# Start of an attention and mixture-of-experts kernel: where the rows of sums are made, how a third slot gets its constant rows, and when a gate split is issued

## The reference

```python
# attention: batch 2, heads 8, sequence 576, head size 64
scores = scale * q @ k.T
cum = cumsum(maximum(s, 0))
bias = -(cum[..., :, None] - cum[..., None, :])
scores = where(causal, -1e9, scores + minimum(bias, 0))
attn = softmax(scores);  x = attn @ v            # -> 1152 tokens x 512
# mixture 1: top 2 of 8 experts, noisy gate; h = relu(x @ w1[e]); out += weight * h @ w2[e]
# mixture 2: all 8 experts, weights balanced by 8 row/column normalisations
```

## Time and profile before

| | us |
|---|---|
| median of 3 runs | 1206.88 (1205.94 to 1207.20) |
| the profiled execution, its own time | 1204.84 |
| its span, first to last instruction | 1203.1 |
| PE busy | 1188.2 |
| mean granted clock | 0.993 |

### The profile page before, as it was taken

One profiled execution on the slowest core, in us unless ns is written; L12 is line 12 of the kernel. 1 busy time (PEld: TensorE's weight loads), 2 busy tenths in 40 slices (PEclk: granted clock), 3 DMA queues, 4 the chain that ended last, 5 costly groups with the idle time before them and its releaser, 6 DMA issues.

```text
span 1203.1 us, 20068 instructions
## 1 busy us (share of the span) xinstructions
PE 1188.2 (99%) x7085; PEld 1062.0 (88%) x7085; DVE 697.3 (58%) x1584; ACT 426.4 (35%) x918; POOL 254.8 (21%) x303
## 2 busy tenths in 40 slices
PE   8999999999999999999999999999999999999998
PEld 6999888888888888889889899899899898898997
DVE  6664775554444451657566575575574675665753
ACT  7675344444344241224123232242241241332320
POOL 8767111111111456201001011011010010110110
PEclk9998999999999999999999999999999999999999
DMA  7770654444455420013120220210211201202102
GB/s 179 182 173 4 246 179 153 155 150 153 180 180 203 161 61 1 1 36 106 36 71 6 64 70 0 70 40 30 70 35 35 70 24 46 70 0 70 35 1 78
DMA packets 40230, 102.81 MB, mean 85 GB/s; under 512 B 4750, under 2 KB 23694, under 8 KB 38010
## 3 DMA queue, kind: packets, MB, share of 16 engines
q1 hardware_dynamic: 33722, 85.70, 22.7%
q0 software_dynamic: 3360, 11.01, 3.0%
q10 hardware_dynamic: 3104, 5.54, 1.4%
HBM read 87.82 MB, written 10.30 MB: 82 GB/s over the span
## 4 chain that ended last, share of the span: by engine, by line
PE 95%; DVE 2%; ACT 1%; DMA 1%; issue 1%; POOL 0%; DVEq 0%; POOLq 0%
PE bank L1164 10%; PE bank L1163 10%; PE bank L1162 9%; PE bank L1118 9%; PE bank L1116 9%; PE bank L1117 9%; PE bank L940 5%; PE bank L942 5%; PE bank L941 5%; PE bank L922 5%; PE bank L924 4%; PE bank L923 4%; PE bank L847 3%; PE bank L828 1%; PE bank L792 1%; PE bank L829 1%
## 5 line engine op out<-in xcount | busy, mean ns | idle before, releaser
L1164 PE MATMUL bank<-part2h,partl 128*128 128x512 f32 x504 | 198.6, 394 | 0.0
L1163 PE MATMUL bank<-part2l,parth 128*128 128x512 f32 x504 | 197.6, 392 | 0.0
L761 POOL TENSOR_TENSOR part2l<-raw_part,part2h 128x512 fp32r<-128x512 f32 x56 | 72.4, 1293 | 589.9 <-ACT part2h L1414 589.9
L1162 PE MATMUL bank<-part2h,parth 128*128 128x512 f32 x504 | 195.7, 388 | 0.0
L1886 DVE SCALAR_TENSOR_TENSOR x_sb<-bank,share_now,x_sb 128x512 f32<-128x512 f32 x126 | 94.1, 747 | 159.5 <-PE bank L1164 159.5
L1118 PE MATMUL bank<-x_forms,forml 128*128 128x288 f32 x448 | 132.1, 295 | 0.0
L1116 PE MATMUL bank<-x_forms,formh 128*128 128x288 f32 x448 | 131.9, 294 | 0.0
L1117 PE MATMUL bank<-x_forms,formh 128*128 128x288 f32 x448 | 131.8, 294 | 0.0
L1565 DVE SCALAR_TENSOR_TENSOR hl<-bank,hh 128x336 fp32r<-128x336 f32 (+1 forms) x88 | 45.7, 519 | 131.5 <-ACT hh L1291 131.3
L922 PE MATMUL bank<-xTh,w1h 128*128 128x336 f32 (+1 forms) x352 | 115.9, 329 | 0.7 <-DVE xTl L1545 0.5
L923 PE MATMUL bank<-xTl,w1h 128*128 128x336 f32 (+1 forms) x352 | 113.9, 324 | 0.0
(11 more groups left out here) (244 smaller groups left out, 2464.2 us busy)
## 6 DMA issues: line engine op xcount, KB each, us to landing
raw<-in_w SPq DMA_DIRECT2D x15, 2048.0 KB, 7.7
raw_part<-in_w1b SPq DMA_DIRECT2D x14, 1024.0 KB, 6.0
raw_part<-in_w2b SPq DMA_DIRECT2D x14, 1024.0 KB, 6.1
k_raw<-in_kT SPq DMA_DIRECT2D x16, 288.0 KB, 5.3
y_dram<-x_sb ACTq DMA_DIRECT2D x16, 256.0 KB, 4.4
q_raw<-in_qT SPq DMA_DIRECT2D x8, 288.0 KB, 5.0
q_two<-w2l SPq DMA_DIRECT2D x8, 288.0 KB, 5.8
x_dram<-x_sb SPq DMA_DIRECT2D x1, 2304.0 KB, 9.2
```

The costliest lines, as they stand in the source:

```text
L1162: pe.matmul(dst, parth[:, l, ts], part2h[:, l, :], start=(l == 0), stop=False)
L1163: pe.matmul(dst, parth[:, l, ts], part2l[:, l, :], start=False, stop=False)
L1164: mm = pe.matmul(dst, partl[:, l, ts], part2h[:, l, :], start=False, stop=(l == FL - 1))
```

## The change

1. `s` of batch 1 is also broadcast, to partitions 32 to 63, by a further DMA on ACT's queue. The scan works on 80 rows.
2. The clip and scale moves from DVE to ACT (a Relu with scale), `s_positive` tells DVE.
3. DVE makes high and low row for partitions 0 and 1, 32 and 33, and the 16 sums with one multiply and one multiply-add on 80 rows (`row_low` and `row_sign` choose high or low). Batch 0's rows are written to `k_top[0]` as before; ACT copies batch 1's rows from `cum_l` into `k_top[0]`. `second_cum` goes.
4. Head 1's rows come by four small DMAs from `cum_h` and `cum_l` on the chip, not through DRAM; `load_cum(1)` goes.
5. Slot 2's constant rows are copied from slot 1 by three DMAs (62, 32 and 30 rows of 1152 values). POOL fills `k_top[0]`, `k_top[1]` and `q_top[1]`, ACT only `q_top[0]`. POOL's 2-row fill moves from step 4 to the start.
6. The copy of `rinv` moves from the start to step -1. `load_v(0)` moves behind `double_q(0)`, `load_v(1)` ahead of the copies, `load_cum(2)` behind them.
7. The products on constants: five of 256 columns at the start; 128 columns beside every rough product of the fill.
8. The six operations of the gate split are issued one a step, behind the row maxima of steps 57, 58, 59, 62, 63 and 64.

```diff
@@ block.sync
-            sp.dma_start(cum_s[0:FIRST_ROWS, :], s[0:1, :].to_broadcast([FIRST_ROWS, S])).then_inc(s_loaded, 16)
+            sp.dma_start(cum_s[0:BATCH_ROWS, :], s[0:1, :].to_broadcast([BATCH_ROWS, S])).then_inc(s_loaded, 16)
...
+            def second_head_cum(row, part):
+                for b in range(B):
+                    at = FIRST_ROWS + B + b
+                    sp.dma_start(k_top[1][row:row + 1, b * S:(b + 1) * S].bitcast(F32), part[at:at + 1, :].bitcast(F32)).then_inc(cum_loaded[1], 16)
+
+            def copy_rows(to, rows):
+                sp.dma_start(to[2][rows, :].bitcast(F32), to[1][rows, :].bitcast(F32)).then_inc(rows_copied, 16)
...
-            load_v(0)
             double_q(0)
-            load_cum(1)
+            load_v(0)
             double_q(1)
             sp.wait_ge(low, LOWS)
             load_raw(2)
+            load_v(1)
+            sp.wait_ge(q_rows_ready, 2)
+            copy_rows(k_top, slice(HD + 2, P))
+            copy_rows(q_top, slice(HD, ROWS_ROUGH))
+            copy_rows(q_top, slice(ROWS_ROUGH + 2, P))
             load_cum(2)
-            load_v(1)
             load_v(2)
@@ block.gpsimd
-            for w in range(HEADS_RING):
-                pool.memset(k_top[w][HD:P, :].bitcast(F32), 1.0).then_inc(aug_ready, 1)
-            pool.memset(q_top[2][HD:P, :].bitcast(F32), 0.0).then_inc(q_rows_clear, 1)
+            for w in range(2):
+                pool.memset(k_top[w][HD:P, :].bitcast(F32), 1.0).then_inc(rows_filled, 1)
+            pool.memset(q_top[1][HD:P, :].bitcast(F32), 0.0).then_inc(rows_filled, 1)
+            pool.wait_ge(rows_filled, 4)
+            pool.wait_ge(q_rows_ready, 1)
+            pool.memset(q_top[1][HD:HD + 2, :].bitcast(F32), 1.0).then_inc(q_rows_ready, 1)
@@ block.tensor
             for _ in range(WARM_UPS):
-                keep_warm(BANK)
+                keep_warm(BANK // 2)
...
-                    keep_warm(BANK // 2 if k < -SCORES_AHEAD else P)
+                    keep_warm(P)
@@ block.scalar
+            act.dma_start(cum_s[BATCH_ROWS:FIRST_ROWS, :], s[1:2, :].to_broadcast([BATCH_ROWS, S])).then_inc(s_loaded, 16)
             act.dma_start(cum_s[CUM_ROWS, :], s).then_inc(s_loaded, 16)
             act.wait_ge(const_ready, 5)
             act.copy(ident_r[:], ident[:]).then_inc(ident_rounded, 1)
+            act.wait_ge(s_loaded, 48)
+            act.activation(cum_p[0:CUM_END, :], cum_s[0:CUM_END, :], ACT.Relu, scale=SQRT_D).then_inc(s_positive, 1)
...
+            act.wait_ge(cum_low, 1)
+            act.copy(k_top[0][HD:HD + 2, S:N], cum_l[BATCH_ROWS:BATCH_ROWS + 2, :].bitcast(F32))
             act.copy(k_top[0][0:HD, S:N], k_raw[0:HD, 0, S:N])
@@ block.vector
-            link(v.tensor_copy(rinv[:].rearrange("p a b -> p (a b)"), ones[:, 0:2 * STEPS]))
-            v.wait_ge(s_loaded, 32)
-            link(v.tensor_scalar(cum_p[0:CUM_END, :], cum_s[0:CUM_END, :], 0.0, SQRT_D, ALU.max, ALU.mult))
+            v.wait_ge(s_positive, 1)
             v.tensor_tensor_scan(cum_s[0:CUM_END, :], cum_p[0:CUM_END, :], zeros_g[0:CUM_END, :], 0.0, ALU.add, ALU.add).then_inc(cum_summed, 1)
             v.wait_ge(cum_summed, 1)
-            link(v.tensor_scalar(cum_p[0:2, :], cum_s[0:2, :], ident[0:2, 1:2], None, ALU.mult))
+            link(v.tensor_scalar(cum_p[0:CUM_END, :], cum_s[0:CUM_END, :], row_low[0:CUM_END, 0:1], None, ALU.mult))
...
-            v.tensor_tensor(cum_l[CUM_ROWS, :], cum_s[CUM_ROWS, :], cum_h[CUM_ROWS, :].bitcast(F32), ALU.subtract).then_inc(cum_low, 1)
+            v.scalar_tensor_tensor(out=cum_l[0:CUM_END, :], in0=cum_h[0:CUM_END, :].bitcast(F32), scalar=row_sign[0:CUM_END, 0:1],
+                                   in1=cum_p[0:CUM_END, :], op0=ALU.mult, op1=ALU.add).then_inc(cum_low, 1)
...
-                if k == GATES_AT:
-                    split_gates()
+                if k == -1:
+                    link(v.tensor_copy(rinv[:].rearrange("p a b -> p (a b)"), ones[:, 0:2 * STEPS]))
+                if k in GATES_AT:
+                    split_gates(GATES_AT.index(k))
```

More of the change, by code:

```diff
@@ L156, in build @@
         row_sign = sb("row_sign", [P, 1], where=attn)
+        row_low = sb("row_low", [P, 1], where=attn)
         attn.close()
@@ L204, in build @@
         s_loaded = sem("s_loaded")
+        s_positive = sem("s_positive")
+        rows_copied = sem("rows_copied")
         cum_summed = sem("cum_summed")
@@ L383, in build @@
         HIGH_AHEAD, LOW_AHEAD = 19, 14
[L384 removed]
+        W1_LOW_AT, EARLY_AT, GATES_AT = ALL - 4 * DC, ALL - ST, (57, 58, 59, 62, 63, 64)
         EARLY = ST
[L386 removed]
+        BATCH_ROWS = 32
+        FIRST_ROWS = B * BATCH_ROWS
         CUM_END = FIRST_ROWS + G
         CUM_ROWS = slice(FIRST_ROWS, CUM_END)
[L389 removed]
+        SECOND_LATER = 2
         FIRST_LOWS = (0, 1, 4, 5, 2, 3, 6, 7)
@@ L484, in _ @@
             sp.wait_ge(cum_high, 1)
-            sp.wait_ge(aug_ready, 2)
-            second_cum(HD, cum_h)
+            sp.wait_ge(rows_filled, 3)
+            second_head_cum(HD, cum_h)
             sp.dma_start(cum_rows[:, 0, :], cum_h[CUM_ROWS, :].bitcast(F32)).then_inc(cum_stored, 16)
             sp.wait_ge(cum_low, 1)
-            second_cum(HD + 1, cum_l)
+            second_head_cum(HD + 1, cum_l)
             sp.dma_start(cum_rows[:, 1, :], cum_l[CUM_ROWS, :].bitcast(F32)).then_inc(cum_stored, 16)
+            double_q(0)
             load_v(0)
-            double_q(0)
-            load_cum(1)
             double_q(1)
@@ L1232, in _ @@
             act.copy(ident_r[:], ident[:]).then_inc(ident_rounded, 1)
+            act.wait_ge(s_loaded, 48)
+            act.activation(cum_p[0:CUM_END, :], cum_s[0:CUM_END, :], ACT.Relu, scale=SQRT_D).then_inc(s_positive, 1)
             act.wait_ge(const_ready, 6)
             act.wait_ge(first_rows, 1)
-            for w in range(2):
-                act.activation(q_top[w][HD:P, 0:S], causal[HD:P, 0:S], ACT.Relu, bias=row_ones[HD:P, 0:1], scale=0.0)
-                act.activation(q_top[w][HD:P, S:N], causal[HD:P, 0:S], ACT.Relu, bias=row_ones[HD:P, 0:1], scale=0.0).then_inc(q_rows_ready, 1)
+            act.activation(q_top[0][HD:P, 0:S], causal[HD:P, 0:S], ACT.Relu, bias=row_ones[HD:P, 0:1], scale=0.0)
+            act.activation(q_top[0][HD:P, S:N], causal[HD:P, 0:S], ACT.Relu, bias=row_ones[HD:P, 0:1], scale=0.0).then_inc(q_rows_ready, 1)
             act.wait_ge(cum_summed, 1)
@@ L1516, in token_low, with split_gates @@
                                 xTh[:, :, ts].bitcast(F32), ALU.subtract).then_inc(st.xTl_ready, 1)
-            def split_gates():
-                v.wait_ge(gates_loaded, 48)
-                for which, (cn, c0, g0) in enumerate(((2 * E, 0, 0), (E, 2 * E, 4 * E))):
-                    high, low = gate_w[:, :, g0:g0 + cn], gate_w[:, :, g0 + cn:g0 + 2 * cn]
+            def split_gates(step):
+                which, part = divmod(step, 3)
+                cn, c0, g0 = ((2 * E, 0, 0), (E, 2 * E, 4 * E))[which]
+                high, low = gate_w[:, :, g0:g0 + cn], gate_w[:, :, g0 + cn:g0 + 2 * cn]
+                if step == 0:
+                    v.wait_ge(gates_loaded, 48)
+                if part == 0:
                     link(v.tensor_copy(high, gates[:, :, c0:c0 + cn]))
+                elif part == 1:
                     link(v.tensor_tensor(low, gates[:, :, c0:c0 + cn], high.bitcast(F32), ALU.subtract))
+                else:
                     link(v.tensor_tensor(fold[which][:], ident[0:2 * cn, 0:cn], ident[0:2 * cn, cn:2 * cn], ALU.add))
-                assert count[0] == GATES_SPLIT, count[0]
+                assert step < 5 or count[0] == GATES_SPLIT, count[0]
             for k in range(-ROUGH_AHEAD, ALL):
```

32 lines of the change are left out of this document (13 added, 19 removed).

## The result

The changed kernel is slower: 1222.91 us median of 6 runs (1212.31 to 1224.63) beside 1206.41 (1204.83 to 1207.72) for the kernel before, ratio 1.0116 with an interval of 1.0075 to 1.0157 (it is taken over all runs, so it isn't the quotient of the two medians). The forecast was 1200.6, with 1197.5 to 1205.3 as its range. The profiled execution of after took 1212.31 us, span 1210.6, so it is 7.5 us longer than the profiled one of before, and it is the shortest of the six. The other five took 2.9 to 12.3 us more, at a mean granted clock of 0.980 to 0.988 against its 0.993; they have no trace, so where they lost that isn't shown.

The account below looks back on a forecast made before the run. The prediction took PE as the bound (busy 1188.2 of 1203.1 us). Head 2 0.8, gate pause 1.1 and clock 4.4 summed to 6.3 us, taking the median from 1206.88 to 1200.6, range 1197.5 to 1205.3.

Parts of the forecast that it names:

- the start: Start of the fill: sums ready sooner, first rough product near 7.7 against 9.10, 1.4 us earlier.
- the dearer case: Start of the fill: DVE's multiply comes behind POOL's 2-row fill, rows ready at 8.2, 0.9 us gained instead of 1.4.
- the overhang at head 2: Copy traffic ahead of head 2's k that can't be hidden: 0.6 to 1.2 us of 2.5 to 3.2.
- The hole: Nearly empty DMA queue from 24.0 to 25.5 us, taken to hide about 1.7 to 2 us of the copies.
- the 0.8: Gain taken at head 2, between 1.4 with the copies free and 0.2 with all of the overhang paid.
- rival 3: Copies and v 2 delay head 2's k and the clock falls: 1212.0 at worst, needing two independent misfortunes; chance 0.07.
- The gate split: Last heads of attention: six operations issued one a step remove PE's pause of 1.09 us, gaining 1.1 us.
- The 4.4 behind it: Half clock from about 100.0 to 110.2 us, taken to go with the gate split's pause: 4.4 us gained.
- rival 1: Clock at the last heads falls all the same, from light work or a moved pause: 1205.0; chance 0.19.
- Rival 2: Head 2 comes late, copies overhang fully, and the clock falls there, losing 1.7 to 3.4 us: 1203.5; chance 0.16.
- Rival 4: Sums stay as late as now, the fill gives 0: 1201.4; 0.58 is its chance together with the forecast.
- The fall at 142 in before: Later clock fall behind a window with 0.6 us idle; could come or go by about 1.7 us.

Follow-up runs that it names:

- experiment 2: The changed kernel run again, unchanged, beside the kernel before on one chip: 1218.66 us, ratio 1.0101.
- Experiment 3: The changed kernel with the 62-row copy cut into 48 and 14 rows and the 30-row one into 16 and 14: 1205.76 us, ratio 1.0048.
- experiment 6: The changed kernel with copies of 30, 32, 32 and 30 rows, moved ahead of the second copy of q: 1207.31 us, ratio 1.0025.
- experiment 7: The changed kernel without its three copies, GpSimd filling slot 2 at steps 0, 2 and 4, `load_cum(2)` behind `load_v(2)`: 1204.79 us, ratio 1.0041.
- experiment 8: The changed kernel without its three copies, VectorE filling slot 2's constant rows in its own gaps: 1197.78 us, ratio 0.9974.
- experiment 4: The probe: kernel before plus four copies (64, 62, 32, 30 rows) near 98 us, each waited for; 62 rows took 7 us at 40 GB/s.
- experiment 5: The kernel before plus three copies of 60, 57 and 58 rows, each waited for: inside 2 us, 4.5 us and 6.5 us.
- experiment 1: The kernel before with only slot 2's constant rows taken from the three copies instead of GpSimd's fills: 1218.74 us, ratio 1.0111.

## Why the prediction was wrong

**The bound and the start were right.** First rough product at 7.46 (forecast 7.7). The sums come as worked out from the rows:

```profile
4.09 1.35 DVE L1469 TENSOR_TENSOR_SCAN cum_s<-cum_p,zeros_g 80x576 f32<-80x576 f32 x1 [0.41 <-ACT cum_p L1244]
5.47 0.52 DVE L1471 TENSOR_SCALAR cum_p<-cum_s,row_low 80x576 f32<-80x576 f32 x1
```

The scan was forecast for 4.4 to 5.8, and DVE's multiply takes 0.52 beside POOL's fill, so the dearer case didn't come. `scores(0)` moved by 1.13 us (14.99 against 16.12), not by 1.8. PE's products are as long as at half clock until about 11 us in this execution (0.74 us for the first rough product, where 0.71 at 36.40 goes with 0.50), although the window's granted clock reads 1.00 there. That isn't the reason, though: in experiment 2's trace they have full length (0.48), and `scores(0)` still comes at 14.80. There and in experiments 3, 6, 7 and 8 PE waits 0.55 to 0.70 us just ahead of it for ACT to place the row maxima, which the prediction hadn't in its chain. Without the copies head 2 comes 1.13 us earlier (26.71), near the 1.4 that I gave for copies that are free. Between executions with the new start the first rough product comes at 7.46 to 8.19, so these tenths aren't firm.

**The step that failed is the overhang at head 2.** I priced 571 KB of copies at the queue's rate of 179 to 225 GB/s, found 2.5 to 3.2 us of traffic, hid most of it in a hole, and took 0.6. Three things were wrong with that.
- *The rate wasn't one for 62 rows.* 62 rows go to two engines, 31 each, 143 KB in a row at some 20 GB/s, 7 us; the 64-row copy of experiment 4, on all engines, took about 1.5. A later copy that needs all engines needs those two as well: k's copy lands at 36.2, when only two engines are still at work. Experiment 3 against after gives the size: 6.27 us at head 2 (36.40 against 30.13), 6.9 in the landing. Nothing in the trace of before shows such a DMA; its large transfers (256 KB and more) have 64 or 128 rows. The place where it stood to be read is the page of the Trainium skill that is named at experiment 5.
- *The hole wasn't free.* Even in good pieces the traffic costs 3.42 us at head 2 (30.13 against 26.71 without copies): 1.66 us because k's copy is issued later (25.07 against 23.41), 1.8 because it lands later (4.9 against 3.1). I had counted the hole at 24 us as room for 1.7 to 2 us, though by its own bounds, 24.0 to 25.5, it holds 1.5, and k's copy has to move in it too. (The landing of 27.1 that I wrote would also give a gain of 0.6; the 0.8 goes with 26.9.)
- *The copy of k no longer waits for ACT, but for SP.* In my chain ACT's rounding of k releases it. Without the copies that is so: rounded at 23.38, issued at 23.41. In after ACT is done at 23.28, 0.1 us earlier, but SP is still issuing what stands ahead, without a break, and comes to k's copy at 24.40, 0.99 us late:

```profile
22.61 0.67 ACT L1219 CAST w2h<-k_raw 128x576 fp32r<-128x576 f32 x1
```
```profile
23.06 0.63 SPq L461 DMA_DIRECT2D v_sb<-in_v_rows  x1
23.73 0.63 SPq L462 DMA_DIRECT2D v_sb<-in_v_tail  x1
```

The three issues cost SP 3.68 us, which I had put at nothing, and the one of `load_cum(2)` behind them takes 1.41 instead of 0.44.

Together that is 9.69 us at head 2 (36.40 against 26.71: 0.99 of issue and 8.7 of landing), against 0.6.

**The clock behind a new wait** was in rival 3 at 4.4 us and measured 4.45 (interval 11.03 against 6.58). In six executions PE was short of work at head 2 or just before (longest pause 10.04, 11.16, 11.16, 3.06, 1.38 and 0.99 us), and each has a loss of 4.1 to 5.6 us ("next" 10.6 to 12.2, against 6.5 to 6.6 in the others).

**Rival 3 was the right one,** with a chance of 0.07: the copies with v 2 delay the copy of k past its present landing, at the worst by 1.8 us. Its mechanism and its place are right, its price was a fifth of the real one, and it ended at 1212.0 where the median is 1222.91. That the profiled execution has 1212.31 is luck: it is the shortest of six, and the rival's sum kept a fall of 4.4 at the end that after doesn't have. I needed "two independent misfortunes" for it; they aren't independent, since the wait brings the fall.

**The gate split was right in mechanism, wrong in what it is worth.** The pause of 1.1 goes in every trace: "end" is 14.2 to 14.5 us in all eight traces with splits one a step, 15.5 to 15.6 in four with splits together. The 4.4 behind it is real (20.24 against 15.52 to 15.59: 4.7; in the probe 6.3), but only in two of the six traces with splits together. So rival 1, that the fall has another cause than the pause, is half true, for this place: no execution fell there without the pause, and most didn't fall with it. What decides isn't settled by these runs. I had charged the fall of one profiled execution to all of them. This fits with experiment 8, whose first turn is 7.4 us ahead of the first trace of before, while its median is only 2.7 us ahead of before's beside it. How many executions of before had the fall is not shown: beside the changed kernel its six times (1204.83 to 1207.72) all lie above its medians beside experiments 3 and 8 (1200.37 and 1200.52).

The Trainium skill's rule in "TensorE: Matmul & The Clock Gate", "Why this matters for your kernels", that I had set aside, warns only of longer idle gaps. The traces stand between: at the splits, pauses of 1.06 to 1.14 us are followed by no fall four times and by one twice.

**The rest.** Rival 2 (clock falls at head 2) is what experiments 6 and 7 ran into. Rival 4 is out by the scan at 4.09. The last mix was to be near 113; the first turn, its neighbour, came at 122.76 instead. The fall at 142 in before isn't in after, as I had allowed for. Of the 16.5 us between the medians the traced execution explains 7.5; the rest lies in executions without a trace, whose mean clock is lower, and its cause stays open.

## What to carry to other kernels

Before pricing a DMA at the queue's rate, factor its row count: here counts that have no large divisor up to 16 went to few engines, and what stood behind waited for those. Count the issuing queue's own time as well, and ask whether it becomes what the next copy waits for. In a fill that is full, constants are better made by a compute engine that has gaps there, sized from its own timeline (here VectorE, 1.02 us each; GpSimd had none). A clock fall seen in one profiled execution is worth its price times the share of executions that have it: look at a second trace of the unchanged kernel before counting on it.

## What the runs showed of the hardware

- A copy between on-chip tiles of 62 rows of 4.5 KB takes 7 us on two of sixteen DMA engines (0.12, 40 GB/s), one of 64 rows about 1.5 us (0.88, 184 GB/s from 98 to 99 us). 57 rows: 4.5 us on three. 60 rows: within 2 us.
- SP's issue of a DMA, mostly 0.44 to 0.64 us, stretched to 1.4 to 1.5 us each while the copies were under way (two in 2.92 us, one in 1.41).
- At half clock PE was busy all the time for 9.5 us in after (36.4 to 46) before the clock came back, and for over 20 us in experiment 6.
- VectorE's fill of 64 rows by 1152 values takes 1.02 us, GpSimd's 1.05.
- VectorE's clip of 48 rows took 1.27 us beside GpSimd's fills (4.54 to 5.81) and 0.45 behind their end (experiment 1).
